# An eighth column for the softmax's constant, and the last edge rows of x in transfers of 16 and 15 rows

## What is computed

```python
w = exp(weight_gen - max(weight_gen, axis=-1, keepdims=True))   # 4 x 4096 tokens, 8 heads, K = 7
w = w / (sum(w, axis=-1, keepdims=True) + 1e-09)
x_pad = concatenate([zeros((B, 6, 192)), x], axis=1)            # six rows of zeros ahead of each batch
x_unf = x_pad[:, arange(S)[:, None] + arange(7)[None, :], :]    # each token sees itself and six before it
out = einsum('bshk,bskhg->bshg', w, x_unf.reshape(B, S, 7, 8, 24))
h = out.reshape(B * S, 192) @ w_in                              # 192 -> 2048
g = s * maximum(h, 0) ** 2 + b
return g @ w_out                                                # 2048 -> 192
```

## Time and profile before

| | |
|---|---|
| median of 3 runs | 1143.09 us (1141.62 to 1144.4) |
| the profiled execution, whole | 1143.53 us |
| span of that execution in the trace | 1141.8 us |
| PE busy | 1131.2 us, 99% of the span |
| DVE busy | 917.2 us, 80% |
| ACT busy | 721.5 us, 63% |
| POOL busy | 121.4 us, 11% |

### The profile page before, as it was taken

The page is one execution under the profiler, slowest core; times in us unless marked ns, Lnnn a source line. Parts: engine busy times, 40 slices in busy tenths (PEclk is TensorE's granted clock), DMA queues, the critical chain, the costliest instruction groups (busy, mean ns, idle before and its releaser), DMA issues.

```text
span 1141.8 us, 31594 instructions
## 1 busy us (share of the span) xinstructions
PE 1131.2 (99%) x12976; PEld 1047.3 (92%) x12976; DVE 917.2 (80%) x1100; ACT 721.5 (63%) x745; POOL 121.4 (11%) x74
## 2 busy tenths in 40 slices
PE   8999999999999999999999999999999999989998
PEld 7999999999999999999999999999999999989997
DVE  8898887778787778877787877788777878777834
ACT  7777656666665566566666655665666666555663
POOL 1100011110111100111101111101111011110111
PEclk9999999999999999999999999999999999999999
DMA  8512334434334333234343343342343433333121
GB/s 254 92 53 66 93 90 107 117 73 108 80 89 117 95 86 105 75 106 117 73 108 80 89 117 90 91 106 74 105 117 74 107 80 89 89 105 102 35 59 29
DMA packets 97820, 106.76 MB, mean 94 GB/s; under 512 B 7336, under 2 KB 77876, under 8 KB 97792
## 3 DMA queue, kind: packets, MB, share of 16 engines
q1 hardware_dynamic: 94960, 103.90, 34.8%
q0 software_dynamic: 2512, 2.26, 1.3%
q10 hardware_dynamic: 320, 0.20, 0.1%
HBM read 70.62 MB, written 35.39 MB: 93 GB/s over the span
## 4 chain that ended last, share of the span: by engine, by line
PE 92%; DMA 3%; issue 2%; DVE 1%; SPq 1%; ACT 1%; POOL 0%; POOLq 0%; ACTq 0%; DVEq 0%
PE hp L1042 44%; PE op L1080 33%; PE op L1089 15%; DMA x_in<-zeros 2%; DVE scratch L641 1%; DMA xT2s<-x_bounce 0%; DMA x_bounce<-x_parts 0%; SPq L268 0%; ACT scratch L462 0%; DMA w_in<-in_weight_gen 0%; SPq L266 0%; POOL scratch L418 0%; POOL scratch L422 0%; SPq L300 0%; SPq L292 0%
## 5 line engine op out<-in xcount | busy, mean ns | idle before, releaser
L1080 PE MATMUL op<-wo,g_hi 64*128 64x384 f32 x4096 | 595.3, 356 | 0.2
L1089 PE MATMUL op<-wo,g_lo 64*128 64x192 f32 x4096 | 529.2, 247 | 0.0
L462 ACT ACTIVATE scratch<-hp 128x1024 f32<-128x1024 f32 x254 | 255.7, 1019 | 381.6 <-PE hp L1042 379.6
L759 DVE TENSOR_TENSOR g_lo<-scratch,g_hi 128x1024 fp32r<-128x1024 f32 x255 | 324.1, 1272 | 187.6 <-ACT g_hi L473 183.4
L1089 PEld LDWEIGHTS op<-wo,g_lo 64*128 64x128 f32 x4096 | 407.4, 188 | 4.4
L1080 PEld LDWEIGHTS op<-wo,g_hi 64*128 64x128 f32 x4096 | 400.2, 184 | 5.0 <-issue 0.3
L1042 PE MATMUL hp<-xT1s,w_hi 64*128 64x512 f32 x2048 | 324.6, 390 | 2.6 <-DMA xT1s<-x_bounce 2.0
L466 ACT ACTIVATE scratch<-scratch 128x1024 f32<-128x1024 f32 x255 | 269.9, 1059 | 6.0
L1042 PEld LDWEIGHTS hp<-xT1s,w_hi 64*128 64x128 f32 x2048 | 189.8, 185 | 30.6 <-DMA xT1s<-x_bounce 2.2
L1042 PE MATMUL hp<-xT1s,w_lo 64*128 64x512 f32 x1024 | 206.4, 392 | 0.0
L672 DVE TENSOR_TENSOR tap<-x_in,w_soft 128x768 f32<-128x768 f32 x186 | 177.4, 954 | 3.2
(11 more groups left out here) (83 smaller groups left out, 272.0 us busy)
## 6 DMA issues: line engine op xcount, KB each, us to landing
x_in<-in_x SPq DMA_DIRECT2D x29, 960.0 KB, 4.9
x_bounce<-x_parts SPq DMA_DIRECT2D x116, 192.0 KB, 3.7
xT1s<-x_bounce SPq DMA_DIRECT2D x29, 512.0 KB, 3.9
xT2s<-x_bounce SPq DMA_DIRECT2D x58, 256.0 KB, 4.9
out<-scratch SPq DMA_DIRECT2D x124, 96.0 KB, 1.8
w_in<-in_weight_gen SPq DMA_DIRECT2D x32, 112.0 KB, 2.1
wo_raw<-in_moe_w_out SPq DMA_DIRECT2D x4, 384.0 KB, 7.7
wo_sums<-in_moe_w_out POOLq DMA_DIRECT2D x4, 384.0 KB, 6.6
```

What stands on the lines that cost most here:

```text
L462: nc.scalar.activation(r[:, b, :], hp[:, PAIR * b:PAIR * (b + 1), :], ACT.Relu).then_inc(relu_done, 1)
L759: nc.vector.tensor_tensor(g_lo[:, buf, tiles, :], pair, g_hi[:, buf, tiles, :].bitcast(F32), ALU.subtract).then_inc(g_lo_ready, 1)
L1080: nc.tensor.matmul(op[:, t, 0:2 * D], g_hi[rows[h], g % 2, j, t * P:(t + 1) * P], wo[rows[h], k, :, :].rearrange("p a d -> p (a d)"), star ...
L1089: mm = nc.tensor.matmul(op[:, t, 0:D], g_lo[rows[h], g % 2, j, t * P:(t + 1) * P], wo[rows[h], k, 0, :], start=False, stop=(k == FT - 1 an ...
```

## The change

Three things are changed. (1) The table of exponentials gets an eighth column, which holds the constant 1e-9; POOL writes it once. The sum runs over eight columns and the addition at L628 goes. (2) Each transfer of 31 edge rows becomes one of 16 and one of 15 rows, so a block has 12 edge transfers and no longer 8. (3) The wait for the edge rows and the transfer of the rest of the tile become a function of their own, called behind the next bounce.

```diff
-        w_exp = sb("w_exp", [P, STEP * H, K])
+        w_exp_eps = sb("w_exp_eps", [P, STEP * H, K + 1])
+        w_exp = w_exp_eps[:, :, 0:K]
...
-        w_eps_added = sem("w_eps_added")
+        eps_ready = sem("eps_ready")
...
                 for q in range(B):
                     a = q * batch_rows
-                    sp.dma_start(x_in[a + 1:a + batch_rows, block, 0:missing, :],
-                                 x_rows[a:a + batch_rows - 1, (TOK - missing) * row:TOK * row]).then_inc(x_edge_loaded[block], FETCH)
+                    for first, n in ((a + 1, batch_rows // 2), (a + 1 + batch_rows // 2, batch_rows // 2 - 1)):
+                        sp.dma_start(x_in[first:first + n, block, 0:missing, :],
+                                     x_rows[first - 1:first - 1 + n, (TOK - missing) * row:TOK * row]).then_inc(x_edge_loaded[block], FETCH)
                     sp.dma_start(x_in[a:a + 1, block, 0:missing, :].rearrange("p t d -> p (t d)"),
                                  zeros[q:q + 1, 0:missing * row]).then_inc(x_edge_loaded[block], FETCH)
-                sp.wait_ge(x_edge_loaded[block], 2 * B * FETCH)
+
+            def load_rest_of_x(block):
+                missing = PAD - STEP * block
+                sp.wait_ge(x_edge_loaded[block], 3 * B * FETCH)
                 sp.dma_start(x_in[:, block, missing:, :], x_rows[:, 0:STEP * (block + 1) * row]).then_inc(x_loaded[block], FETCH)
...
             edge_loads(STEPS - 4, 0)
             bounce(STEPS - 3, 1)
+            load_rest_of_x(0)
             store(STEPS - 5)
             edge_loads(STEPS - 3, 1)
             bounce(STEPS - 2, 0)
+            load_rest_of_x(1)
             store(STEPS - 4)
...
                                     base=0, pattern=[[-1, P]], channel_multiplier=1).then_inc(ident_ready, 1)
+            nc.gpsimd.memset(w_exp_eps[:, :, K:K + 1], EPS).then_inc(eps_ready, 1)
             nc.gpsimd.memset(zeros[:, :], 0.0).then_inc(zeros_ready, 1)
...
-                nc.vector.reduce_sum(w_sum[:, :], w_exp[:, :, :], AX_X).then_inc(w_sum_ready, 1)
+                nc.vector.reduce_sum(w_sum[:, :], w_exp_eps[:, :, :], AX_X).then_inc(w_sum_ready, 1)
                 dve.wait_ge(w_sum_ready, i + 1)
-                nc.vector.tensor_scalar_add(w_sum[:, :], w_sum[:, :], EPS).then_inc(w_eps_added, 1)
-                dve.wait_ge(w_eps_added, i + 1)
                 nc.vector.reciprocal(w_rec[:, :], w_sum[:, :]).then_inc(w_rec_ready, 1)
...
             shift_weights(0)
+            dve.wait_ge(eps_ready, 1)
             normalise_weights(0)
```

## The result

| | before | after |
|---|---|---|
| median | 1143.57 us (1141.62 to 1145.0, 12 runs) | 1146.33 us (1145.71 to 1146.47, 12 runs) |
| ratio | 1 | 1.0019 (95% interval 1.0012 to 1.0027) |
| span of the profiled execution | 1141.8 us | 1144.5 us |

The changed kernel is 2.8 us slower, where 5.5 us less were forecast. What was forecast for step 29 came as forecast; two other things took it back and more. Lines of the code have moved by up to 8: L1042 is now L1049, L672 is L678, L752 is L758, L759 is L765.

A forecast was written before the change was run, and what follows sets the result against it. PE was taken to bound the steady steps. Removing a 5.31 us stall and 0.19 us in the first step, 5.5 us together, took the median from 1143.09 to 1137.6 us, range 1135.8 to 1139.8.

The forecast's parts named there:

- the stall of step 29: PE's late first product at 1036.55 instead of 1031.24; issuing the bounce before the edge-row wait was to save 5.31 us.
- both waits: PE's waits in the late stretch, 1.96 us for xT1s and 1.41 us for xT2s, both forecast to go.
- the low clock: Granted clock of 0.81 in PE's late stretch, costing 1.94 us through slower matmuls; forecast to go with the waits.
- the steady beat: PE's first products 8.72 us apart in the steady steps, claimed to be PE's own and untouched by the change.
- Rival (c): Slower: the gapped table makes DVE and ACT instructions dearer every step, 1153 us at 2 us more per step; chance 0.04.
- The rest of x: Remaining tile transfer, issued later behind xT2s; its lateness was to cost 0, range 0 to +1 us.
- The split, 0: Edge rows in 16 and 15: four more issues per block, 2 us of SP in a pause, costing nothing.
- The eighth column, -0.19 us: DVE's dropped addition less a longer sum, gaining 0.19 us in the first step only, bounds 0 and -0.22.
- Rival (a): Split edge rows land no sooner, as if one engine still carried them; 1139.8 us, chance 0.07.
- Rival (b): No gain: ACT, DVE or the late rest of x holds PE at 1022.5 as long; 1142.9 us, chance 0.07.

The follow-up runs named there:

- e3: The kernel before with edge rows in transfers of 16 and 15, SP's old order and seven columns; 1138.34 us.
- e1: The kernel before with 128 unused bytes per partition behind the table of exponentials, no instruction changed; 1148.33 us.
- e2: The changed kernel with the eight-column table behind all other tensors and 896 unused bytes in its old place; 1141.71 us.
- e5: The changed kernel with SP's old order and the eight-column table behind all other tensors; 1138.28 us.
- e4: The kernel before with the wait and the rest of x behind the bounce, edge rows still in transfers of 31; 1147.43 us.
- e7: The kernel before with 128 unused bytes ahead of g_hi, moving g_hi, g_lo and scratch but not xT; 1141.8 us.
- e12: e5 with 128 unused bytes ahead of g_hi, moving g_hi, g_lo and scratch; 1136.51 us.

## Why the prediction was wrong, point by point

**"-5.31 us" for the stall of step 29: the size was right, the credit was not.** The bounce left SP when its input was there, both waits and the low clock went, and e3, with a beat of 8.72 throughout, puts the worth of an undisturbed end at 5.1 us. But e3 has that without the reordering to which I gave it.

**"More cannot come from here, since the steady beat on both sides is PE's own": this failed, by 4.6 to 4.9 us.** The sentence took the beat as a constant of PE's instructions. It also depends on the place of their operands, and the eighth column moved these by 128 bytes: 4.9 us by e1 against before, 4.6 by the changed kernel against e2. I worked out the column from its own instructions alone and never asked what stands behind it in memory. Rival (c) came close in form, a small price in every step, but named the wrong mechanism: the gapped table costs nothing (L628 takes 0.39 us as before).

**The rest of x, "I take 0, with a range of 0 to +1": this failed, measured +3.4 us** (e2 against e5). Block 0 behaved as reckoned: DVE waited 2.15 us, within the 3.35 that I said the place bears. The 3.35 counted only DVE and ACT. POOL's additions start behind the second tap, and the later they start the longer they stand beside DVE's rounding. The sign was in the trace of before. There, too, the tap had waited 1.90 us, and the rounding behind it is long:

```profile
1023.00 2.29 DVE L752 CAST g_hi<-scratch 128x1024 fp32r<-128x1024 f32 x1
```

PE, standing still for xT at that moment, felt nothing of it. That stall was DVE's cover; I removed it and kept the bill at zero. For block 1 the error adds up: x_parts was ready at 1046.97, 1.6 us later than four beats of 8.76 behind the 1010.31 of the step before, the rest of x took 6.2 us to land and not 4.9, and the wait was 4.58 us and not 1.5 to 3. The last two intervals come from there.

**The split, 0: wrong in what it was credited with.** I gave the whole gain to the order and called the split a condition. By e3 and e4 it is the split that brings it, and the order gives part back.

**The eighth column, -0.19 us: 0.10 measured.** The addition went and the sum grew by 0.03 as worked out; the wait ahead of it grew by 0.08, which I had put at nothing.

**Rival (a)**, one engine still carrying the edge rows, is the case of e4, whose edge rows stay in transfers of 31. I had 1139.8 us for it; with this order it is 1147.4. The landing at 1023 to 1024 was nearly right (1024.4), but the wait of PE is 4.16 us and not 1 to 2, and as much again goes with it, most of it at the low clock. **Rival (b)** named ACT or DVE as what could hold PE next; DVE did, though not at 1022.5 but from 1044 on, and for 3 us, not for the whole gain.

**The chances.** 0.04 for slower hung on one mechanism inside DVE's instructions. A change that reaches into every one of 127 groups through the allocation was not among the cases. The range was also added up loosely: 1137.6 - 1.5 and 1137.6 + 1.3 + 1 are 1136.1 and 1139.9, not 1135.8 and 1139.6; 1146.33 lies far outside either.

## What to carry to other kernels

When an edit changes the size of a buffer, list what is allocated behind it and keep those addresses (put the new buffer last, or pad), or price the beat as unknown: here 128 bytes cost 4.6 to 4.9 us of 1143 and a chosen pad gave 1.8. Before counting a removed stall as gain, look at what else was late beside it, above all instructions that took longer than their median there: a stall on the bottleneck hides lateness on every other engine. And if a slow transfer is spread so that it lands early, leave its follower in front; moving it back as well only makes it late again.

## What the runs showed of the hardware

The time of this kernel's matmuls in a full pipeline depends on the place of their operand in SBUF: with xT 192 bytes behind a multiple of 1024 a first product of 36 pairs takes 4.16 us, at 0 and 256 it takes 4.20, at 320 4.22 to 4.23. With g at 320 instead of 192 a group takes 8.707 us for 8.72 in e7 and 8.69 in e12's profiled run, where the second product takes 4.53 for 4.56. Why is not known. DMA: 31 rows went at 27 GB/s and a share of one sixteenth; those in transfers of 16 and 15 had landed 1.5 us behind the end of the last issue and 8 us behind the first (e3). A bounce queued behind the 31-row transfers took 6.05 us to issue for 2.6 (e4), and the last edge transfer there, a row of zeros, 5.01 us for 0.5; that a loaded engine holds up the issuing queue fits this and was not tried apart. And a vector instruction and POOL's additions, side by side, each take longer: 2.34 for 0.69 us and 2.65 for 1.85 (e2).
